# Attention with a learned bias and a gated feed-forward on one core: bias stores split over two DMA queues, their rows reordered, two value loads moved

## The reference

```python
scores = scale * np.matmul(q, k.transpose(0, 1, 3, 2))      # B,H,S,D = 4,8,576,64
psi_rel = np.log1p(np.abs(rel))                              # rel = pos_i - pos_j
psi_i = np.log1p(np.maximum(pos[:, None], 1.0))
h = np.maximum((psi_rel / psi_i)[..., None] @ w1 + b1, 0.0)  # 32 hidden units
bias = h @ w2                                                # S x S x 8 heads, same for all batches
scores = scores + bias.transpose(2, 0, 1)[None]
attn = softmax(scores);  attn_out = attn @ v
x = attn_out as [2304, 512]
out = (sigmoid(x @ w_gate) * (x @ w_val)) @ w_out            # 512 -> 1536 -> 512
```

## Time and profile before

| | us |
|---|---|
| median of 3 runs (lowest, highest) | 814.01 (813.38, 817.22) |
| the profiled execution | 812.84 |
| its span in the trace | 811.1 |
| PE busy | 769.7 (95%) |
| ACT busy, DVE busy, POOL busy | 344.8, 349.8, 195.0 |

### The profile page before, as it was taken

The page is one execution under the profiler, slowest core; times in us unless marked ns, Lnnn a source line. Parts: engine busy times, 40 slices in busy tenths (PEclk is TensorE's granted clock), DMA queues, the critical chain, the costliest instruction groups (busy, mean ns, idle before and its releaser), DMA issues.

```text
span 811.1 us, 13830 instructions
## 1 busy us (share of the span) xinstructions
PE 769.7 (95%) x5296; PEld 637.6 (79%) x5296; DVE 349.8 (43%) x845; ACT 344.8 (43%) x684; POOL 195.0 (24%) x363
## 2 busy tenths in 40 slices
PE   5666899999999999999899999999999999999998
PEld 2222677777777777689879998999899899989996
DVE  6885777777777777624321221122022212211220
ACT  6775766767667676632321221222122112212210
POOL 0000567647555446768200000000000000000000
PEclk9988999999999999999999999999999999999999
DMA  5769333342332332223322000100100020000001
GB/s 134 164 154 194 87 93 86 77 119 70 82 87 71 84 87 65 56 82 88 114 78 65 1 1 27 53 1 1 48 31 1 14 65 1 1 26 14 1 1 39
DMA packets 86336, 49.92 MB, mean 62 GB/s; under 512 B 60160, under 2 KB 79744, under 8 KB 86272
## 3 DMA queue, kind: packets, MB, share of 16 engines
q1 hardware_dynamic: 86272, 49.05, 23.4%
HBM read 28.98 MB, written 9.44 MB: 47 GB/s over the span
## 4 chain that ended last, share of the span: by engine, by line
PE 84%; DMA 5%; ACT 4%; DVE 2%; SPq 2%; POOL 2%; issue 1%; DVEq 0%; POOLq 0%; ACTq 0%
PE f_ps L1048 18%; PE g_ps L996 16%; PE u_ps L996 15%; PE v_ps L976 11%; PE so_ps L911 8%; PE ty_ps L924 4%; PE tx_ps L937 3%; PE so_ps L856 2%; DMA x_raw<-in_w_out 2%; PE so_ps L906 2%; DMA bias<-bias_rows 2%; ACT bias_rows L582 1%; PE tx_ps L954 1%; POOL w L525 1%; PE ty_ps L879 1%
## 5 line engine op out<-in xcount | busy, mean ns | idle before, releaser
L996 PE MATMUL g_ps<-x_h,w 128*128 128x384 f32 x576 | 147.3, 336 | 3.4 <-DVE hid L825 3.4
L996 PE MATMUL u_ps<-x_h,w 128*128 128x384 f32 x576 | 146.8, 335 | 0.0
L825 DVE TENSOR_TENSOR hid<-u_ps,sig 128x384 f32<-128x384 f32 x72 | 40.1, 557 | 239.8 <-PE u_ps L996 239.8
L615 ACT ACTIVATE probs<-neg_scores,neg_max 128x576 f32<-128x576 f32 x144 | 111.1, 771 | 60.3 <-DVE neg_max L749 60.3
L508 POOL TENSOR_SCALAR probs<-probs,recip 128x512 f32<-128x512 f32 x128 | 89.1, 696 | 172.0 <-DVE recip L769 172.0
L996 PEld LDWEIGHTS g_ps<-x_h,w 128*128 128x128 f32 x576 | 104.4, 188 | 4.5 <-DVE hid L825 3.8
L996 PEld LDWEIGHTS u_ps<-x_h,w 128*128 128x128 f32 x576 | 104.5, 189 | 0.5 <-issue 0.5
L681 ACT ACTIVATE h_h<-hid 128x384 fp32r<-128x384 f32 x72 | 37.9, 526 | 149.4 <-DVE hid L825 149.4
L996 PE MATMUL g_ps<-x_l,w 128*128 128x384 f32 x288 | 96.7, 336 | 0.0
L996 PE MATMUL u_ps<-x_l,w 128*128 128x384 f32 x288 | 96.4, 335 | 0.0
L749 DVE CUSTOM_DVE_ANT_0 neg_scores<-so_ps,bias 128x576 f32<-128x576 f32 x128 | 91.9, 755 | 3.3 <-PE so_ps L911 3.2
(11 more groups left out here) (87 smaller groups left out, 1163.1 us busy)
## 6 DMA issues: line engine op xcount, KB each, us to landing
bias<-bias_rows SPq DMA_DIRECT2D x16, 576.0 KB, 5.7
x_raw<-attn_transposed SPq DMA_DIRECT2D x6, 768.0 KB, 4.7
out<-out_sb SPq DMA_DIRECT2D x18, 256.0 KB, 2.0
q_raw<-in_q SPq DMA_DIRECT2D x32, 128.0 KB, 2.5
k_raw<-in_k SPq DMA_DIRECT2D x32, 128.0 KB, 2.6
v_main<-in_v SPq DMA_DIRECT2D x32, 128.0 KB, 2.3
w_raw<-in_w_gate SPq DMA_DIRECT2D x12, 256.0 KB, 2.9
w_raw<-in_w_val SPq DMA_DIRECT2D x12, 256.0 KB, 2.9
```

The lines of the kernel that those rows point to most:

```text
L615: nc.scalar.activation(probs[s % RING][:, place, :], neg_scores[:, place, :], ACT.Exp, bias=neg_max[:, stat(s, place)], scale=-1.0, accum_ ...
L825: nc.vector.tensor_tensor(hid[f % 2][:, :], u_ps[f % 3][:, 0:CH], sig[f % 2][:, :], ALU.mult).then_inc(gated, 1)
L996: last = nc.tensor.matmul(bank[f % 3][:, 0:CH], w[:, f, part, i, t, :], x[:, t, :], start=m == 0, stop=m == len(terms) - 1)
```

## The change

Three things are changed in the bias stage and at its end.

`duo(d)` gives the first row of a pair. Before, successive pairs take rows 0, 1, 2, ..., 7 of each eight. Now they take 0, 4, 1, 5, 2, 6, 3, 7 (`GRP` is 4). The pairs of the last 64 rows stay as they are. `base_row`, from which the features' windows are computed, follows `duo`.

The stores of pairs 1, 3, 5, 7, 11, 13, 15 and 17 are issued by ACT on its own DMA queue, each behind `relu_feats` and ahead of `copy_bias` of the next even unit, and the last one behind the loop. SP keeps pairs 0, 2, 4, 6, 10, 12, 14, 16 and the tails' 8 and 9.

The eight loads of v for the first two pairs of heads stood between SP's stores of pairs 11 and 12, and 13 and 14. Now they stand at steps 0 and 2 of the attention.

```diff
 def duo(d):
-    if d < ROW_STEP:
-        return 0, d
-    if d < ROW_STEP + TAIL_DUOS:
+    if ROW_STEP <= d < ROW_STEP + TAIL_DUOS:
         return NT, 2 * (d - ROW_STEP)
-    return 2, d - ROW_STEP - TAIL_DUOS
+    t, n = (0, d) if d < ROW_STEP else (2, d - ROW_STEP - TAIL_DUOS)
+    return t, n // 2 + n % 2 * GRP
...
+        def stored_by_act(d):
+            return duo(d)[0] < NT and d % 2 == 1
...
             def store_bias(d):
+                if stored_by_act(d):
+                    return
                 i = d % ROW_BUFS
                 sp.wait_ge(bias_copied, 2 * d + 2)
...
-                if d == DUOS - 6:
-                    load_v(0)
-                if d == DUOS - 4:
-                    load_v(1)
...
             for s in range(STEPS + DRAIN):
                 pair, m = divmod(s, SPP)
+                if s in (0, 2):
+                    load_v(s // 2)
...
+            def store_bias(d):
+                i = d % ROW_BUFS
+                t, at = duo(d)
+                act.wait_ge(bias_copied, 2 * d + 2)
+                act.dma_start(bias[at::ROW_STEP, :, t:t + 2, :], bias_rows[i][:, :, :]).then_inc(bias_stored[i], 16)
...
                 if u + 1 < UNITS:
                     relu_feats(u + 1)
+                if u % 2 == 0 and u and stored_by_act(u // 2 - 1):
+                    store_bias(u // 2 - 1)
                 copy_bias(u)
+            store_bias(DUOS - 1)
```

## The result

| | us |
|---|---|
| before, median of 15 runs | 813.96 |
| changed, median of 15 runs | 810.49 |
| ratio | 0.9945, 95% interval 0.9929 to 0.9961 |
| profiled execution, before and changed | 812.84 and 808.04 |
| span, before and changed | 811.1 and 806.2 |

The ratio is worth 0.55%, about 4.5 us (the medians differ by 3.5), under half of the 9.7 forecast and outside the range. The bias stage ends when PE starts its first score matmul, at 78.55 us before and 73.2 us now. Of the 5.3 us gained there the span keeps 4.9.

The account below looks back on a forecast made before the run. The bias stage was taken to wait for stores that SP issues late. From the floor's gain, 12.3 - 0.3 - 1.2 - 0.3 - 0.8 = 9.7 us less, predicting 804.0 us, range 800.8 to 809.5.

Parts of the forecast that it names:

- Order of the rows: Bias stage stores with alternating rows: the sum needs only that they aren't slower than now, 5 us against 6.6.
- Rival 1: Bias stage: the transfers remain the bound; 9.0 to 4.3 us less, the middle 6.7 giving 807.3; 18 in 100.
- Pair 5 on ACT's queue: Bias stage, ahead of unit 16: issued at about 29.4, lands at 34.5 to 35.5, before 35.88.
- Odd pairs in general: Bias stage: pair 7 and later odd ones have no loads ahead; from pair 11 every store has at least 6 us.
- The v loads: Moved from ahead of pairs 12 to 14 to steps 0 and 2: cost nothing; uncovered, eight issues would be 5 us.
- The engines' floor: Bias stage, units 15 to 35: 29.4 us of paces plus 1.7, unit 35 at 65.5; at most 12.3 us to gain.
- The preparation ahead of unit 18: Bias stage, second preparation (q alone), PE turning q behind unit 17: adds 1.7 us, bounds 0.7 and 2.7.
- ACT's issues: Eight store issues on ACT: 0.1 us each, 0.8 in all; upper bound 0.56 each, 4.5 us.
- Rivals 2 and 3: ACT's issues: 2, paid in full, 808, 12 in 100; 3, 2.13 us each time, about 816, 4 in 100.
- The tails: Bias stage, unit 24: pair 9, issued by SP, lands after unit 24 is wanted; 1.2 us charged (0.6 and 1.8).
- The stage's end: Step 2 shift, waiting for pair 17's store: a landing of 5 to 6 us stays hidden with 1 to 2 left.

## Why the prediction failed

- **The step that failed** stands under "Order of the rows": "In the sum I need only that stores aren't slower than now: 5 us against 6.6." I took the landing of a lone store, issued at once, for every store behind unit 15, and so charged nothing for pair 5, 0.3 us for pair 6 and nothing from pair 11 on. They are not alone. Of ACT's 6.2 us of waits 3.7 stand at units 16 and 18, for pairs 5 and 6, whose packets shared the DMA engines with q, k and each other (share 1.03 from 34 to 45 us), 0.3 at unit 24 and 2.2 from unit 26 on. There a pair's first copy stands at 57.94, 61.90, 65.05, 68.17 and 71.05, 3.28 us apart in the mean against a floor of 2.94. 576 KB at 208 GB/s are 2.8 us, so a backlog once made, by the loads or the tails, is worked off by only 0.1 us a pair. Half the bytes removed all waits for stores with issue order and queues unchanged, which shows the transfers' own time as the cause.
- **What that makes of the sum**: from the copy of unit 15 to that of unit 35 the kernel before takes 43.4 us, the forecast was 33.7, the changed kernel took 36.7. So 3.0 of the 9.7 us are missing there, the failed step net of the other terms. A further 1.3 went ahead of unit 15 in this execution (PE's clock, 0.93), and 0.4 behind the stage. How much of the 4.5 us of the ratio each makes up in the mean of all runs isn't known.
- **Rival 1** was the right one: 4.3 to 9.0 us less, middle 6.7, which is what came from unit 15 to 35; that it is met so closely is luck, since its data was to end by 79.1 and ended at 79.8. I gave it 18 in 100 although already showed 1.01 and 198 GB/s, and SP's late issue had the place of the main cause.
- **Pair 5 on ACT's queue**: forecast to land at 34.5 to 35.5. Issued at 30.63, it held unit 16 until 39.07, 8.4 us. The queue was free, the engines were not; before, 5.2 us passed from a later issue (34.04) to the same moment.
- **Odd pairs in general**: 8.0 us to land in the median against 5.3 on SP. The rule of the Trainium skill, "DMA: Bandwidth & Descriptors", section "Issuing engines are not separate DMA queues", that queues share the 16 DMA engines and only issue time is saved, holds here: alone, the second queue gave 0.3%, and beside the moved v loads nothing that shows.
- **The v loads**: I priced their removal at nothing of its own and only let the delay of pairs 12 to 14 go. Moved alone they give 0.9937, all of the gain. They took SP's time (from 57.3 to 61.2 and from 62.6 to 67.5 us) and the engines' (576 KB, as much as one store) at the place where both were short; which of the two counted for more wasn't tried.
- **The engines' floor** of 31.1 us from unit 15 to 35 was right. With half the bytes on two queues it took 32.85, of which 1.72 are the wait for the tails: 31.1, with PE's clock at 1.00 all through. With half the bytes on one queue unit 35 came at 67.4, with four buffers at 68.0, 1.9 to 2.5 us behind the 65.5, and in both PE was granted the lower clock for a part (0.95 in the mean from 34 to 68 us), and the first has 0.8 us of waits for transfers besides. The preparation ahead of unit 18 was right too: units 17 to 20 took 6.2 us with half the bytes, 1.8 more than three paces (forecast 1.7).
- **ACT's issues**: 0.8 us forecast, nothing measured (0.54 to 0.62 us each, under a feature instruction). Rivals 2 and 3 are out.
- **The tails**: 1.2 us at unit 24 forecast, 0.3 in the changed kernel, where unit 24 was late itself, 1.7 in the run with half the bytes, and 0.4 in the same on one queue.
- **The stage's end**: "it stays hidden with 1 to 2 us left" failed: 0.8 us of wait at step 2, and 2.2 with four buffers. Pair 17's store, issued at 73.20, was taken to land in 5 to 6 us; step 2 waited for it until 80.97, 7.8 us. What the copies gain beyond the transfers' pace is given back there.
- **The rows**: the sum used nothing of them. The runs show the part of the Trainium skill's rule ("SBUF — State Buffer", section on the DMA port swizzle) that concerns one store: a store into 16 neighbours moves 115 GB/s, one into rows 8 apart 208. The skill's ports (4 and 8 of 16 reached) would give 109 and 217 by its 435 GB/s, an estimate that fits both within 6 in 100. But the earlier trace rows was misread for it: 197 GB/s is the mean of a window of 3 us, of which the lone store's packets filled 2.55, so while it ran it moved 231 GB/s, more than the stores in a row and more than the estimate. Alternating the halves brought little: over pairs 11 to 16 a packet took 354 ns in the mean in the changed kernel and 362 with the old rows; on one queue it was 349 (four buffers, v later) and 364 (v alone, old rows). In the time nothing shows (0.9989, interval over 1). Two stores seldom used both halves at once: from 60 to 75 us packets of both queues' stores were under way together in 25% of the time, and for the rest one queue's alone.

## What to carry to other kernels

When a producer waits for its transfers, compare the interval between transfers with what each keeps the engines busy in a row, not the allowed latency with a lone landing. Where the share was at 1.0 here, a second queue and an earlier issue mostly moved the wait; taking other traffic out of the stretch cut it, and fewer bytes removed it. More buffers removed it too, and moved it to the reader. And ask what waits for the last transfer: a stage that ends sooner than its stores can land gives the difference back at the next reader. Before two single profiles are compared, compare a stretch that the change doesn't touch; here it differed by up to 1.8 us.

## What the runs showed of the hardware

- SBUF to SBUF stores of 576 KB: 208 GB/s into 16 partitions 8 apart, 115 GB/s into 16 neighbours, in both cases with the DMA engines' share at 1.03 to 1.04. A full share doesn't say what the engines can move.
- Reading the same bytes from device memory instead of SBUF left the rate of stores in a row at 210 GB/s.
- A DMA issue on ACT (0.55 us) ran beside an instruction already started; ACT's pace of 1.47 us per unit didn't change.
- The kernel before and the run with v alone have the same instructions up to pair 11. From 9.5 to 34.5 us PE's granted clock was 1.00 in the one and 0.93 in the other, and unit 15 was copied 1.1 us later in the latter (34.41 and 35.48).
